# Scores of a token with itself by an elementwise product and a matmul with ones, in a gated linear attention kernel

## The chip, the cores and the metric

The kernel runs on one core of a Trainium2 chip. Its time is the device time of one execution in microseconds (us), the median of several runs. The core's engines are TensorE (PE, and PEld for its loading of stationary weights), VectorE (DVE), ScalarE (ACT), GpSimd (POOL) and SyncE (SP), each working through a list of its own in the order in which the program gives it, with semaphores between them.

## The reference

Inputs: q, k, v, f_logit of shape 4 x 8 x 768 x 48 (batch, heads, tokens, width), and the weights of two feed-forward parts. All of it is fp32.

```python
f = 1.0 / (1.0 + np.exp(-f_logit))
for t in range(S):
    state = f[:, :, t, :, None] * state + np.einsum('bhd,bhe->bhde', k[:, :, t], v[:, :, t])
    y[:, :, t] = np.einsum('bhd,bhde->bhe', q[:, :, t], state)
```

The output of this attention (8 heads side by side, 768 tokens x 384) goes through a low-rank mix over the tokens and `u + relu(u @ w_ch1) @ w_ch2` (first part), and then `h = relu(x @ w_in)`, a gated convolution over three tokens, and `@ w_out` (second part).

In a block of 64 tokens, the attention is a matrix of scores. The score of query token t with key token s up to t is the sum over the 48 channels of q[t] k[s] and of the gates of the tokens s+1 to t. With itself (s = t) a token has no gate: the score is q[t] . k[t].

## The kernel before

The unit of the attention is a duo: 256 tokens of one batch, all 8 heads, held as channels x tokens in `q_t`, `k_t` and `gates` (112 partitions: one head of a pair in rows 0 to 47, the other in 64 to 111; 1024 columns). There are three duos for each of the 4 batches, 12 in all. A duo's scores are 32 blocks of 64 x 64.

Scores are made in seven steps. `DIAG` comes first: 32 matmuls of k with q (line 547), each in one quadrant of the array (the pair `par`, `ch`), of which only the diagonal is kept: VectorE copies it under `diag_mask` into `scores` (line 949). Between, VectorE multiplies the whole of q by the gates (line 991). Then come levels 0 to 5. Level l gives the scores of query tokens whose bit l is one with key tokens whose bit l is zero, in the same group of 2 x 2^l tokens: 32 matmuls with 32 moving columns (line 566), and a masked copy (line 955, `take_scores`; ScalarE does it in the last levels). After its matmuls, a level multiplies half of q by products of gates on VectorE (line 1002) and half of k on GpSimd (line 1123, at level 0 by the gates themselves). GpSimd also makes the products of gates for levels 1 and 2 (line 1126, `pairs_ready`), VectorE the later ones. Steps T, U and Y close a duo: transposed k, the update of the state, the output, copied to `x` by ScalarE.

A list written out by `schedule()` sets the order on each engine. The three duos of batch 0 run first, interleaved among themselves, each with its own buffers, before any feed-forward work: I call this the prologue (0 to about 81 us). After it the duos of batch b+1 are spread over the 40 slots of the feed-forward work of batch b, one step a slot at first. A slot of the first part (0 to 23) holds `first1` (nine matmuls, lines 681 to 683), the step of a duo, and `second1` (nine matmuls, lines 700 to 705) of two slots before; slots 0 and 1 have no `second1`, but transposes and mix matmuls (lines 660 and 666). DIAG stands in slots 0, 11 and 22, level 0 in 1, 12 and 23. In a slot's list, the residual of `first1` (`r_lo`, line 1044, on VectorE) stands ahead of the duo's step. In batch 0's slots GpSimd also splits the weights (line 1133), two pieces a slot, ahead of the duo's step.

## Time and profile before

| | before |
|---|---|
| median of 3 runs | 738.42 us (738.24 to 738.48) |
| profiled execution | 738.63 us, of which its span is 736.7 us |
| PE busy | 704.6 us, 96% of the span |
| PEld busy | 664.4 us |
| DVE busy | 441.7 us |
| ACT busy | 246.4 us |
| POOL busy | 289.7 us |

The span is from the first to the last instruction of the profiled execution; 1.9 us of its time lie around it. An engine is busy while an instruction of its own runs. A row of the timeline gives start and duration in us, engine, line, operation, what is written and what is read, and how many instructions were merged (x64); in brackets the idle time of the engine before it and who ended it. A fp32 matmul is two records of the trace: line 547 has 32 matmuls and x64 in a duo. The time from one record's start to the next one's is shorter than a record, since they are pipelined.

### The profile page before, as it was taken

How to read it: one execution, taken by the hardware profiler on the slowest of the kernel's cores; microseconds unless marked ns; L12 is line 12 of the kernel's file. 1: busy time of each engine (PE TensorE's matmuls, PEld its weight loads, DVE VectorE, ACT ScalarE, POOL GpSimd, SP SyncE). 2: the span in 40 equal slices, each digit the busy share in tenths (PEclk: the TensorE clock that was granted, in tenths of full speed). 3: DMA queues.
4: the chain of work that ended last, by engine and by line, in shares of the span. 5: the costliest groups of instructions: out<-in, count | busy, mean ns of one | idle time of the engine just before them, and what ended most of it. 6: DMA issues, size and time to landing. Idle time of an engine off the chain costs nothing.

```text
span 736.7 us, 23832 instructions
## 1 busy us (share of the span) xinstructions
PE 704.6 (96%) x10748; PEld 664.4 (90%) x10748; DVE 441.7 (60%) x706; ACT 246.4 (33%) x504; POOL 289.7 (39%) x262
## 2 busy tenths in 40 slices
PE   3888989999999999999999999999999999999998
PEld 3787789989999899999999889999999889999997
DVE  6895474573898464464598655365489832121875
ACT  1034524342236322212245431213134542121453
POOL 4862597691453234062253225145055311030432
PEclk9999999999999999999999999999999999999999
DMA  8331353412001110100201200110000000000000
GB/s 202 100 91 40 109 148 91 127 57 66 24 3 54 45 55 23 46 24 24 67 2 46 53 34 25 41 49 24 23 2 2 34 33 1 1 1 0 1 33 32
DMA packets 24293, 33.75 MB, mean 46 GB/s; under 512 B 5152, under 2 KB 17184, under 8 KB 24192
## 3 DMA queue, kind: packets, MB, share of 16 engines
q1 hardware_dynamic: 23184, 30.46, 15.3%
q10 hardware_dynamic: 1008, 1.77, 1.0%
q8 instruction: 84, 1.38, 0.8%
q14 instruction: 17, 0.14, 0.1%
HBM read 27.50 MB, written 4.72 MB: 44 GB/s over the span
## 4 chain that ended last, share of the span: by engine, by line
PE 72%; DVE 18%; issue 4%; ACT 3%; POOL 1%; DMA 1%; ACTq 0%; DVEq 0%; POOLq 0%
PE acc L700 8%; PE hb L681 7%; PE att L566 7%; PE hb L682 7%; PE hb L683 6%; PE acc L701 6%; PE acc L705 6%; DVE conv L1074 5%; DVE q_t L1002 3%; PE att L612 3%; DVE conv L1071 3%; PE acc L739 2%; PE hb L649 2%; PE acc L740 2%; DVE conv L1058 2%
## 5 line engine op out<-in xcount | busy, mean ns | idle before, releaser
L1044 DVE SCALAR_TENSOR_TENSOR r_lo<-hb,r_hi 128x386 fp32r<-128x386 f32 (+1 forms) x96 | 53.5, 557 | 193.2 <-ACT r_hi L864 193.2
L864 ACT ACTIVATE r_hi<-hb 128x386 fp32r<-128x386 f32 (+1 forms) x96 | 47.2, 492 | 260.1 <-PE hb L683 260.1
L1160 POOL TENSOR_TENSOR r_lo<-conv,r_hi 128x384 fp32r<-128x384 f32 x64 | 61.7, 964 | 168.6 <-ACT r_hi L879 168.6
L700 PE MATMUL acc<-r_hi,w_ch_hi 128*128 128x386 f32 (+1 forms) x288 | 103.8, 360 | 0.0
L1123 POOL TENSOR_TENSOR k_t<-k_t,blocks 112x512 f32<-112x512 f32 x60 | 81.5, 1361 | 55.2 <-PE att L566 45.0
L681 PE MATMUL hb<-u_hi,w_ch_hi 128*128 128x386 f32 (+1 forms) x288 | 98.3, 341 | 0.2 <-DVE r_lo L1044 0.2
L682 PE MATMUL hb<-u_hi,w_ch_lo 128*128 128x386 f32 (+1 forms) x288 | 97.5, 339 | 0.0
L701 PE MATMUL acc<-r_hi,w_ch_lo 128*128 128x386 f32 (+1 forms) x288 | 97.3, 338 | 0.0
L683 PE MATMUL hb<-u_lo,w_ch_hi 128*128 128x386 f32 (+1 forms) x288 | 96.9, 337 | 0.0
L566 PEld LDWEIGHTS att<-q_t,k_t 48*64 48x64 f32 (+3 forms) x3840 | 59.3, 134 | 25.6 <-issue 23.9
L1074 DVE SCALAR_TENSOR_TENSOR conv<-hb,convw,conv 128x384 f32<-128x384 f32 x128 | 79.1, 618 | 4.5
L1123 POOL TENSOR_TENSOR k_t<-k_t,gates 112x512 f32<-112x512 f32 x12 | 23.3, 1942 | 140.5 <-PE att L566 140.2
L566 PE MATMUL att<-q_t,k_t 48*64 48x32 f32 (+3 forms) x3840 | 66.0, 219 | 11.3 <-DVE scores L949 3.4
L1002 DVE TENSOR_TENSOR q_t<-q_t,blocks 112x512 f32<-112x512 f32 x60 | 68.3, 1138 | 7.2 <-PE att L566 5.0
L739 PE MATMUL acc<-w_out_hi,r_hi 128*128 128x384 f32 x192 | 67.6, 352 | 1.3 <-ACT ostage L902 1.3
L705 PE MATMUL acc<-r_lo,w_ch_hi 128*128 128x386 f32 (+1 forms) x288 | 66.1, 338 | 0.0
L720 PE MATMUL hb<-u_hi,w_in_hi 128*128 128x388 f32 x192 | 65.4, 341 | 0.0
L722 PE MATMUL hb<-u_lo,w_in_hi 128*128 128x388 f32 x192 | 65.0, 338 | 0.0
L721 PE MATMUL hb<-u_hi,w_in_lo 128*128 128x388 f32 x192 | 64.8, 338 | 0.0
L740 PE MATMUL acc<-w_out_lo,r_hi 128*128 128x384 f32 x192 | 64.7, 337 | 0.0
L700 PEld LDWEIGHTS acc<-r_hi,w_ch_hi 128*128 128x128 f32 x288 | 54.2, 188 | 2.6
L873 ACT ACTIVATE conv<-conv 128x384 f32<-128x384 f32 x64 | 33.7, 527 | 65.3 <-DVE conv L1074 65.3
(134 smaller groups left out, 1343.4 us busy)
## 6 DMA issues: line engine op xcount, KB each, us to landing
v_p<-in_vn_dram SPq DMA_DIRECT2D x12, 384.0 KB, 3.6
out_dram<-ostage SPq DMA_DIRECT2D x24, 192.0 KB, 2.0
q_t<-in_qT_dram SPq DMA_DIRECT2D x21, 192.0 KB, 3.6
k_t<-in_kT_dram SPq DMA_DIRECT2D x21, 192.0 KB, 3.5
gates<-in_fT_dram SPq DMA_DIRECT2D x21, 192.0 KB, 3.5
ostage<-in_w_ch_dram SPq DMA_DIRECT2D x14, 192.0 KB, 2.8
conv<-in_w_ch_dram SPq DMA_DIRECT2D x10, 192.0 KB, 2.9
ostage<-in_w_out_dram SPq DMA_DIRECT2D x5, 192.0 KB, 2.5
```

The source lines that it names most:

```text
L566: mm = pe.matmul(banks[o:o + left, par, g * C:g * C + 32], k[rows, first:first + left], moving, start=True, stop=True, skip_group_check=True)
L681: pe.matmul(o, wh[:, t, ws], u_hi[:, t, cols], start=(t == 0), stop=False)
L682: pe.matmul(o, wl[:, t, ws], u_hi[:, t, cols], start=False, stop=False)
L683: mm = pe.matmul(o, wh[:, t, ws], u_lo[:, t, cols], start=False, stop=(t == CT - 1))
L700: pe.matmul(o, wh[:, j, ws], r_hi[:, s, 0:width], start=(j == 0), stop=False)
L701: pe.matmul(o, wl[:, j, ws], r_hi[:, s, 0:width], start=False, stop=False)
L705: mm = pe.matmul(o, wh[:, j, ws], r_lo[:, s, 0:width], start=False, stop=(j == N1 - 1))
L739: pe.matmul(o, r_hi[:, s, ts], wh[:, j, :], start=(j == 0), stop=False)
L740: pe.matmul(o, r_hi[:, s, ts], wl[:, j, :], start=False, stop=False)
L1002: nc.vector.tensor_tensor(view, view, block_product(products(gates[i], blocks[i], st), c, 0), ALU.mult).then_inc(q_ready, 1)
L1074: nc.vector.scalar_tensor_tensor(out=c, in0=hid[:, tap + 1:HALF + tap + 1], scalar=convw[:, j, tap:tap + 1], in1=c, op0=ALU.mult, op1=ALU. ...
L1123: nc.gpsimd.tensor_tensor(view, view, block_product(ends, c, 1), ALU.mult).then_inc(k_ready, 1)
```

## The change

The step DIAG is replaced by a step EVEN at the same places of the list, with no work on PE.

- EVEN on VectorE: the product of q and k for even tokens alone (512 columns) goes into the unused second half of `blocks`; then q of the even tokens is multiplied by their gates. On GpSimd, the multiplication of k by the gates (before: after level 0's matmuls) and the first products of gates stand here, and wait for that product (`selves_ready`) and the gates.
- Level 0 on PE: first 4 matmuls of ones (48 x 64) with the product, 256 moving columns each, one in each quadrant; they put the sum over the channels in every row of the first 32 columns of a block. Then the 32 matmuls of k with odd q go to the other 32 columns. k is gated by then in its even tokens and q is not yet gated in its odd ones, so that the same matmul gives an odd token's score with itself and with the even token before it.
- Level 0 on VectorE: odd q is multiplied by the products of two gates, and one masked copy of 1024 columns takes all, in place of line 949's (1024) and level 0's of line 955 (512). It reads its source with a step: neighbours in `scores` lie 32 columns apart in PSUM.
- The constants: `ones` is set, and `first_mask` is made in three small steps. The loads of the third duo wait for the even q of the first (`q_ready`) and no longer for `level_done` of DIAG.

```diff
-                if st == DIAG:
-                    pe.wait_ge(loaded_q[q_of(n)], 32 * q_use(n))
-                    pe.wait_ge(loaded_k[i], 32 * set_use(n))
+                if st == EVEN:
+                    return
+                if st == 0:
+                    if n == 0:
+                        pe.wait_ge(ones_ready, 1)
+                    pe.wait_ge(selves_ready, selves(n))
                     if set_before(n) is not None:
                         pe.wait_ge(x_copied, copies(set_before(n)))
...
-                                mm = pe.matmul(banks[o:o + C, par, g * C:(g + 1) * C], k[rows, first:first + C],
-                                               q[rows, first:first + C], start=True, stop=True, skip_group_check=True)
-                    mm.then_inc(level_done, 1)
-                elif st < LEVELS:
+                    sums = self_products(n).rearrange("p (g h m) -> p g h m", h=2, m=32)
+                    for par, ch in QUADRANTS:
+                        rows, o = slice(C * par, C * par + D), C * ch
+                        pe.matmul(banks[o:o + C, par, :].rearrange("p (g x) -> p g x", x=C)[:, :, 0:32], ones[rows, :],
+                                  sums[rows][:, :, ch, :], start=True, stop=True, skip_group_check=True)
+                if st < LEVELS:
                     c = 1 << st
-                    pe.wait_ge(q_ready, levels(n, st - 1))
+                    pe.wait_ge(k_ready, gated(n, max(st - 1, 0)))
                     if st > 0:
-                        pe.wait_ge(k_ready, gated(n, st - 1))
...
             def take_scores(n, st):
...
+                if st == 0:
                     nc.vector.copy_predicated(
-                        sc[:].rearrange("p (g t) -> p g t", t=C),
-                        diag_mask[:].rearrange("p (o t) -> p o t", o=1).broadcast_to([P, BLOCKS, C]),
-                        from_psum).then_inc(level_taken, 1)
+                        sc[:].rearrange("p (g m two) -> p g m two", g=BLOCKS, two=2),
+                        first_mask[:].rearrange("p (o m two) -> p o m two", o=1, two=2).broadcast_to([P, BLOCKS, 32, 2]),
+                        from_psum.rearrange("p g (two m) -> p g m two", two=2)).then_inc(level_taken, 1)
...
-                if st == DIAG:
+                if st == EVEN:
+                    dve.wait_ge(loaded_q[q_of(n)], 32 * q_use(n))
+                    dve.wait_ge(loaded_k[i], 32 * set_use(n))
+                    even, even_k = split_blocks(q, 1)[:, :, 0, 0], split_blocks(k_t[i][0:PR, :], 1)[:, :, 0, 0]
+                    nc.vector.tensor_tensor(self_products(n), even, even_k, ALU.mult).then_inc(selves_ready, 1)
                     dve.wait_ge(gates_ready, n + 1)
-                    dve.wait_ge(level_done, levels(n, DIAG))
-                    nc.vector.tensor_tensor(q, q, gates[i][0:PR, :], ALU.mult).then_inc(q_ready, 1)
+                    dve.wait_ge(selves_ready, selves(n))
+                    nc.vector.tensor_tensor(even, even, split_blocks(gates[i][0:PR, :], 1)[:, :, 0, 0],
+                                            ALU.mult).then_inc(q_ready, 1)
+                elif st == 0:
+
+                    dve.wait_ge(pairs_ready, paired(n, 0))
+                    dve.wait_ge(level_done, levels(n, 0))
+                    odd = split_blocks(q, 1)[:, :, 1, 0]
+                    nc.vector.tensor_tensor(odd, odd, products(gates[i], blocks[i], 1), ALU.mult).then_inc(q_ready, 1)
...
-                pool.wait_ge(level_done, levels(n, st))
                 if st == 0:
+                    pool.wait_ge(selves_ready, selves(n))
                     pool.wait_ge(gates_ready, n + 1)
                 else:
+                    pool.wait_ge(level_done, levels(n, st))
                     pool.wait_ge(k_ready, gated(n, st - 1))
```

VectorE, slots 11 and 12 of batch 1 (the step DIAG or EVEN, then level 0). Before:

```order
266 L991 TENSOR_TENSOR q_t<-q_t,gates 112x1024 [waits level_done,gates_ready]
267 L949 COPY_PREDICATED scores<-diag_mask,att 128x1024
268 L1044 SCALAR_TENSOR_TENSOR r_lo<-hb,r_hi 128x382 [waits r_hi_ready]
269 L1002 TENSOR_TENSOR q_t<-q_t,gates 112x512 [waits q_ready,level_done]
270 L955 COPY_PREDICATED scores<-masks,att 128x512 [waits level_taken]
```

The same place now:

```order
269 L1019 TENSOR_TENSOR blocks<-q_t,k_t 112x512 [waits loaded_k0,loaded_q0]
270 L1022 TENSOR_TENSOR q_t<-q_t,gates 112x512 [waits selves_ready,gates_ready]
271 L1082 SCALAR_TENSOR_TENSOR r_lo<-hb,r_hi 128x382 [waits r_hi_ready]
272 L1029 TENSOR_TENSOR q_t<-q_t,blocks 112x512 [waits level_done,pairs_ready]
273 L976 COPY_PREDICATED scores<-first_mask,att 128x1024
```

The step needs nothing of PE any more, one masked copy is gone, and level 0's multiplication waits for GpSimd's products of gates.

GpSimd at the start of the program, three duos interleaved (the rows with `gates` are the first gating of k and the first products of a duo). Before:

```order
13 L1123 TENSOR_TENSOR k_t<-k_t,gates 112x512 [waits gates_ready,level_done,cleared_k]
14 L1126 TENSOR_TENSOR blocks<-gates 112x512
15 L1123 TENSOR_TENSOR k_t<-k_t,blocks 112x256x2 [waits pairs_ready,k_ready,level_done]
16 L1126 TENSOR_TENSOR blocks<-blocks 112x256
17 L1123 TENSOR_TENSOR k_t<-k_t,gates 112x512 [waits gates_ready,level_done]
18 L1126 TENSOR_TENSOR blocks<-gates 112x512
19 L1123 TENSOR_TENSOR k_t<-k_t,blocks 112x128x4 [waits pairs_ready,k_ready,level_done]
20 L1123 TENSOR_TENSOR k_t<-k_t,blocks 112x256x2 [waits pairs_ready,k_ready,level_done]
21 L1126 TENSOR_TENSOR blocks<-blocks 112x256
22 L1123 TENSOR_TENSOR k_t<-k_t,blocks 112x64x8 [waits merged_ready,k_ready,level_done]
23 L1123 TENSOR_TENSOR k_t<-k_t,gates 112x512 [waits gates_ready,level_done]
```

The same place now:

```order
13 L1163 TENSOR_TENSOR k_t<-k_t,gates 112x512 [waits gates_ready,selves_ready,cleared_k]
14 L1166 TENSOR_TENSOR blocks<-gates 112x512
15 L1163 TENSOR_TENSOR k_t<-k_t,gates 112x512 [waits gates_ready,selves_ready]
16 L1166 TENSOR_TENSOR blocks<-gates 112x512
17 L1163 TENSOR_TENSOR k_t<-k_t,blocks 112x256x2 [waits pairs_ready,k_ready,level_done]
18 L1166 TENSOR_TENSOR blocks<-blocks 112x256
19 L1163 TENSOR_TENSOR k_t<-k_t,blocks 112x128x4 [waits pairs_ready,k_ready,level_done]
20 L1163 TENSOR_TENSOR k_t<-k_t,gates 112x512 [waits gates_ready,selves_ready]
21 L1166 TENSOR_TENSOR blocks<-gates 112x512
22 L1163 TENSOR_TENSOR k_t<-k_t,blocks 112x256x2 [waits pairs_ready,k_ready,level_done]
```

The second duo's pair of instructions moved ahead of the first duo's level 1, the third duo's ahead of the second duo's level 1.

## Rows read from the trace of the kernel before

**Rows 1.** The page: busy time of each engine; TensorE's granted clock, 40 slices.

```profile
PE 704.6 (96%) x10748; PEld 664.4 (90%) x10748; DVE 441.7 (60%) x706; ACT 246.4 (33%) x504; POOL 289.7 (39%) x262
...
PEclk9999999999999999999999999999999999999999
```

**Rows 2.** Waits of PE from 78 us on: total us, times, longest.

```profile
PE att L566 <- DVE scores L955: 2.8, 2, 1.5
PE att L566 <- POOL k_t L1123: 1.4, 3, 0.5
```

**Rows 3.** Timeline of PE, slots 11 to 13 of batch 1.

```profile
306.81 0.34 PE L683 MATMUL hb<-u_lo,w_ch_hi 128*128 128x386 f32 x1
307.08 1.16 PE L547 MATMUL att<-q_t,k_t 48*64 48x64 f32 x64
308.17 0.44 PE L700 MATMUL acc<-r_hi,w_ch_hi 128*128 128x386 f32 x1
308.45 0.34 PE L701 MATMUL acc<-r_hi,w_ch_lo 128*128 128x386 f32 x1
...
311.54 1.14 PE L566 MATMUL att<-q_t,k_t 48*64 48x32 f32 x64
...
315.98 1.14 PE L566 MATMUL att<-q_t,k_t 48*64 48x32 f32 x64
```

**Rows 4.** Timeline of DVE, the same slots.

```profile
307.71 0.56 DVE L1044 SCALAR_TENSOR_TENSOR r_lo<-hb,r_hi 128x386 fp32r<-128x386 f32 x1 [5.12 <-ACT r_hi L864]
308.38 1.23 DVE L991 TENSOR_TENSOR q_t<-q_t,gates 112x1024 f32<-112x1024 f32 x1
309.52 1.31 DVE L949 COPY_PREDICATED scores<-diag_mask,att 128x1024 f32<-128x1024 uint8 x1
...
312.74 0.69 DVE L1002 TENSOR_TENSOR q_t<-q_t,gates 112x512 f32<-112x512 f32 x1
313.35 1.35 DVE L955 COPY_PREDICATED scores<-masks,att 128x512 f32<-128x512 uint8 x1
```

**Rows 5.** Timeline of POOL, the same slots.

```profile
312.79 2.03 POOL L1123 TENSOR_TENSOR k_t<-k_t,gates 112x512 f32<-112x512 f32 x1 [22.54 <-PE att L566]
314.79 1.03 POOL L1126 TENSOR_TENSOR blocks<-gates 112x512 f32<-112x512 f32 x1
```

**Rows 6.** Timeline of PE, the mix matmuls of batch 0.

```profile
77.52 2.82 PE L649 MATMUL hb<-x,mixu 128*96 128x384 f32 x8
80.18 0.60 PE L660 MATMUL hb<-ident_r,x 128*128 128x128 f32 x4
```

**Rows 7.** Timeline of DVE: level 2's masked copy of a duo.

```profile
148.28 0.70 DVE L955 COPY_PREDICATED scores<-masks,att 128x512 f32<-128x512 uint8 x1
```

**Rows 8.** Timeline of PE, slots 0 to 2 of batch 1.

```profile
261.21 1.16 PE L547 MATMUL att<-q_t,k_t 48*64 48x64 f32 x64
...
265.11 1.14 PE L566 MATMUL att<-q_t,k_t 48*64 48x32 f32 x64
...
268.49 1.14 PE L566 MATMUL att<-q_t,k_t 48*64 48x32 f32 x64 [0.47 <-POOL k_t L1123]
```

**Rows 9.** Timeline of DVE: slot 2 of batch 0; then slot 0 of batch 1.

```profile
94.14 3.46 DVE L1002 TENSOR_TENSOR q_t<-q_t,blocks 112x512 f32<-112x512 f32 x1 [0.52 <-PE att L566]
...
262.51 1.23 DVE L991 TENSOR_TENSOR q_t<-q_t,gates 112x1024 f32<-112x1024 f32 x1
```

**Rows 10.** Timeline of all engines in the prologue.

```profile
15.27 1.99 PE L547 MATMUL acc<-q_t,k_t 48*64 48x64 f32 x64
...
24.48 1.50 POOL L1123 TENSOR_TENSOR k_t<-k_t,gates 112x512 f32<-112x512 f32 x1
...
29.16 1.66 POOL L1123 TENSOR_TENSOR k_t<-k_t,blocks 112x512 f32<-112x512 f32 x1 [0.57 <-PE acc L566]
...
33.36 1.54 POOL L1123 TENSOR_TENSOR k_t<-k_t,gates 112x512 f32<-112x512 f32 x1 [0.38 <-PE hb L566]
...
37.82 1.93 PE L566 MATMUL hb<-q_t,k_t 48*64 48x32 f32 x64
```

More of the change, by code:

```diff
@@ L37 @@
 QUADRANTS = [(par, ch) for par in range(2) for ch in range(2)]
-DIAG, T, U, Y = -1, LEVELS, LEVELS + 1, LEVELS + 2
-STEPS = list(range(DIAG, Y + 1))
+EVEN, T, U, Y = -1, LEVELS, LEVELS + 1, LEVELS + 2
+STEPS = list(range(EVEN, Y + 1))
 PAD = 2
@@ L305, in bass_gla_lowrank_mix_ffn_gated_conv_ffn @@
         convw = sb("convw", [P, N2, 3])
+        ones = sb("ones", [P, C])
         ident_r = sb("ident_r", [P, P], F32R)
```

72 lines of the change are left out of this document (42 added, 30 removed).

## The prediction

> **What bounds the kernel now.** I read the page first: PE is busy for 704.6 of 736.7 us [rows 1], so after the prologue a microsecond taken from PE is a microsecond of the time, unless PE then waits for somebody. Next come the waits of PE from 78 us on. Those that touch the steps of this change are small: 2.8 us for VectorE's masked copies and 1.4 us for GpSimd's gating of k, three times up to 0.5 us [rows 2]. The reader is to see two things: PE's own work is the bound, and in slot 2 of a batch the wait for GpSimd is already there. Last come the timelines of the slots that change.
>
> The own time of the profiled execution is 738.63 us, 736.7 of span and 1.9 around it; the sum is made against 738.63, and the median is 0.2 lower. A measurement of this kernel can tell 0.2%, some 1.5 us.
>
> **1. What leaves PE.** DIAG's 64 records start at 307.08, and the next large matmul at 308.17 [rows 3]. The large matmul before started at 306.81, and one follows another in 0.17 to 0.18 us, so PE was free for the next at 306.99: the group takes 1.18 us. The first large matmul behind it takes 0.28 us to the next in place of 0.18 [rows 3], which adds 0.10. A duo so gives back 1.28 us; of nine duos behind the prologue that would be 11.5 us.
>
> **2. What comes to PE.** Four matmuls of 256 columns, eight records. The nearest row is the mix: eight fp32 records of 384 columns start at 77.52, and the next group at 80.18, 0.333 us each [rows 6], so 0.22 us for 256 columns. If the four quadrants run side by side the group takes 2 x 0.22 = 0.44 us, one after another 8 x 0.22 = 1.78. DIAG decides: its 64 records of 64 columns would by the same rate take 64 x 0.055 = 3.5 us one after another, and took 1.16 [rows 3], three at least at a time. So it is between 0.44 and 1.78/3 = 0.59 us; I take 0.45. It stands directly ahead of level 0's small matmuls, so no second change to and from large matmuls is paid.
>
> A rule bears on it: the Trainium skill, page "TensorE: Matmul & The Clock Gate", section "Part 3: Packing small matmuls", has four row-packed tiles run 3.07 times as fast as one by one. By that the group would take 0.58 us, and the nine duos 1.2 us more than my sum where PE is what is late.
>
> **3. The new wait of level 0, slots 11 and 22 (six duos).** Level 0 now waits for GpSimd's gating of k, which waits for VectorE's product. The chain, with the times of rows 4: `r_lo` starts at 307.71 and is over at 308.27; the product of 512 columns is of the kind of the 0.69 us row (512 columns, sources with a step of two), so 308.95. VectorE goes straight on with even q, another 0.69. GpSimd's gating took 2.03 us where VectorE's 0.69 us instruction had started just ahead of it, 312.74 against 312.79 [rows 4, 5], and 1.50 where it had not [rows 10]. The pair of instructions meets in the same way now, so I take 2.03: k is ready at 311.0. PE meanwhile has `second1` and `first1`; before, level 0 started at 311.54 [rows 3], so without DIAG PE gets there at 310.26, does the ones until 310.71, and waits until 311.03. Level 0 starts 0.5 us earlier than before, and not 0.83. Six duos: **-3.0 us**. If GpSimd gets in first (1.50) it is -0.83 each and -5.0; if the ones take 0.59 nothing changes, since k is what is late.
>
> The products of gates end 1.03 us [rows 5] behind the gating, at 312.0, before level 0's matmuls do (312.2): VectorE's new wait for them costs nothing.
>
> **4. The masked copy.** It has 1024 columns, contiguous in the target, as line 949's with 1.31 us [rows 4]. Level 0's old copy took 1.35 us for 512 columns [rows 4], level 2's 0.70 [rows 7]. Mask and source are read alike in both, and only the target differs (single words against runs of four); this penalty goes away. But the new source steps by 32 columns at every element, which no row shows. Bounds: 1.31, and 2.4, twice the rate of 1.31, as the penalty of the target was a factor of two. Nothing excludes either end; I take the middle, 1.85.
>
> The Trainium skill, page "Vector Engine (DVE) Microarchitecture Reference", section "5.2 Measured stream behaviour on trn2", gives 1.73 ns a column where one source hops at every element against 1.054 contiguous. By that the copy takes 1.9 us; no row here shows such a source.
>
> In slots 12 and 23 the copy is hidden: level 0's matmuls end at about 312.1, multiplication and copy take 0.65 + 1.85, so 314.7; level 1 would start at 315.98 [rows 3] less 0.5. Even 2.4 us fit, by 0.2.
>
> **5. Slots 0 to 2 (three duos).** Here no `second1` stands between. In batch 1, VectorE's L991 started at 262.51, held by DIAG [rows 9]; the product can start at 262.35, so k is ready at 262.35 + 0.69 + 0.05 + 2.03 = 265.1. Before, level 0 started at 265.11 [rows 8]. PE would be there at 263.83 + 0.45 = 264.3, and waits: all of step 1 is eaten, gain 0. Its work ends at 266.3. Between it and level 1 stand only `first1`'s 1.6 us, and before, level 1 waited for GpSimd until 268.49 [rows 8]. That wait goes, and VectorE's is next: 266.35 + 0.6 + 1.85 + 0.1 = 268.9, so **+0.45 us** in batches 1 and 2 (-0.1 with 1.31, +1.0 with 2.4): +0.9.
>
> In batch 0, GpSimd's weight pieces lie between. Before, VectorE's multiplication at 94.14 took 3.46 us [rows 9] in place of 0.69, while pieces and gating ran on GpSimd, and level 2 waited for 1.5 us of it [rows 2]. Gating and products now stand two pieces earlier, so about two pieces of work are over before that point. I take back 1.2 of the 1.5 us, less the 0.45: **-0.8** (bounds -1.5 and +1.5, if the new multiplication by the products falls into such a stretch instead).
>
> **6. The prologue.** PE does not bound it; the three engines take turns. There the same L547 group takes 1.99 us, not 1.16 [rows 10, 3], with a granted clock shown as full in both [rows 1]; the ones I put at 0.9. I listed the starts with the rows' durations. First duo: gates at 11.0, GpSimd 2.0, level 0's 1.9 us from 13.0, VectorE 0.7 + copy, level 1 at 17.7 with 1.85. The second duo's pair on GpSimd (1.5 + 1.0) comes ahead of the first's level 1. Further on the third duo's pair, which stood at 33.36, goes ahead of the second's level 1, which stood at 29.16 [rows 10]: that stays where it was (29.4 with a copy of 1.31, 31.2 with 2.4), and GpSimd is free of the pair behind it. The third duo's level 1, before at 37.82 [rows 10], then starts at 35.2 with 1.31, and at 38 with 2.4 at most. With 1.85: **-1.3 us** (+0.3 to -2.6).
>
> **7. What costs nothing.** The loads of the third duo start some 1.5 us later (the even q of the first duo in place of its DIAG), ahead of ACT's second sigmoid and SP's later loads; the third duo's q is first needed at about 27 us. `ones` and the mask steps are 0.5 us of VectorE before the first gates are ready (11.0). If q and k were late, the product would be, by as much.
>
> **Sum:** -3.0 + 0.9 - 0.8 - 1.3 = -4.2; 738.63 - 4.2 = 734.4 us, as a median 734.2.
>
> **The rivals.**
> A. The stepped source is free: copy 1.31. Steps 5 and 6 become -0.2, -1.2 and -2.6, sum -7.0: 731.4. For it: a step of two costs nothing in the 0.69 us rows. Against: these stay within neighbouring words.
> B. The stepped source halves the rate: copy 2.4. Sum -3.0 + 2.0 + 0 - 0.3 = -1.3: 737.1. For it: the factor of two that the masked copy shows at its target.
> C. The chain through VectorE and GpSimd becomes the bound of level 0. Each 0.1 us that it is longer than 2.8 us costs 0.1 in all nine duos. It decides from 0.47 us on (no gain); if GpSimd loses to both new multiplications and not to one, it is 0.69 longer: -4.2 + 6.2 = +2.0: 740.4. For it: the 3.46 us row [rows 9] and the 0.5 us at 312.79. Against: the product must be over before GpSimd may start, so it can meet one only.
> D. Part of the copy's stepped read is far dearer than a factor of two. From 2.65 us it shows in slots 13 and 24 too; slower than before from about 2.9. Taken with C.
>
> **How the numbers follow.** Forecast 0.45, A 0.22, B 0.18, C and D 0.15. The forecast's own range is 732 to 737. With A and B, the ends of steps 5 and 6, the range is 730.5 to 739.5, which leaves C's tail and a luckier GpSimd out. Faster by over 0.2% (under 736.9): 0.9 of the forecast, all of A, a third of B: 0.67. Slower: C and D, 0.15. Within: 0.18.
>
> **What would show it.** The new copy's duration (1.3, 1.85 or 2.4); eight records of ones within 0.45 us; level 0 of slots 12 and 23 waiting 0.3 us for GpSimd's k, of slot 1 some 0.8; level 1 of slot 2 waiting for VectorE's copy; the gating of k at 2.0 or 1.5 us; the end of the prologue's attention 1.3 us earlier. The prediction is wrong if ones run one after another (+1.3 each), if another engine's pace in the prologue undoes its part, or if the copy is outside 1.3 to 2.4.

## The result, and the profile after

Eight executions of the changed kernel have a median of **735.36 us** (733.25 to 737.34), the kernel before on the same chip 738.66 us (736.91 to 742.12): a ratio of 0.9928, interval 0.9906 to 0.9951. That ratio is not the quotient of the two medians, which is 0.9955: by the medians the change is worth 3.3 us, by the ratio some 5.3 (3.6 to 6.9). The forecast was 734.2 us, with a range of 730.5 to 739.5. The profiled execution took 736.56 us, 734.8 of them span, against 738.63 and 736.7 before.

The page of the changed kernel, busy time of each engine and the granted clock in 40 slices:

```profile
PE 699.3 (95%) x10076; PEld 657.7 (90%) x10076; DVE 446.1 (61%) x709; ACT 246.3 (34%) x504; POOL 286.3 (39%) x262
...
PEclk9999979999999999999999999999999999999999
```

PE's busy time fell by 5.3 us [rows 1] and the span by 1.9. The clock row has what the row of before does not: one slice, the sixth, at 7 tenths. The waits of PE from 78 us on (total us, times, longest) are the next thing to read:

```profile
PE hb L700 <- DVE r_lo L1082: 2.9, 2, 2.8
PE att L585 <- DVE scores L976: 1.9, 2, 0.9
...
PE att L585 <- DVE scores L982: 1.3, 1, 1.3
PE att L585 <- POOL k_t L1163: 0.8, 3, 0.5
```

One wait of 2.8 us is new. The waits for masked copies are 3.2 us (1.9 and 1.3) and were 2.8, those for GpSimd's k are 0.8 and were 1.4 [rows 2]. The new wait stands in batch 0, behind level 0 of slot 1 and ahead of the first matmul of slot 2. The timelines of PE, VectorE and GpSimd there (start, duration, and in brackets the idle time before and who ended it):

```profile
87.00 0.66 PE L567 MATMUL att<-blocks,ones 48*64 48x256 f32 x8
88.13 1.14 PE L585 MATMUL att<-q_t,k_t 48*64 48x32 f32 x64 [0.47 <-POOL k_t L1163]
92.05 0.69 PE L700 MATMUL hb<-u_hi,w_ch_hi 128*128 128x386 f32 x1 [2.78 <-DVE r_lo L1082]
92.53 0.53 PE L701 MATMUL hb<-u_hi,w_ch_lo 128*128 128x386 f32 x1
...
95.25 1.93 PE L585 MATMUL att<-q_t,k_t 48*64 48x32 f32 x64
...
102.27 1.14 PE L585 MATMUL att<-q_t,k_t 48*64 48x32 f32 x64
```

```profile
86.60 4.92 DVE L1022 TENSOR_TENSOR q_t<-q_t,gates 112x512 f32<-112x512 f32 x1
91.44 0.55 DVE L1082 SCALAR_TENSOR_TENSOR r_lo<-hb,r_hi 128x386 fp32r<-128x386 f32 x1
```

```profile
86.58 1.50 POOL L1163 TENSOR_TENSOR k_t<-k_t,gates 112x512 f32<-112x512 f32 x1 [0.63 <-DVE blocks L1019]
88.03 1.04 POOL L1166 TENSOR_TENSOR blocks<-gates 112x512 f32<-112x512 f32 x1
89.03 1.95 POOL L1173 TENSOR_TENSOR w_ch_lo<-ostage,w_ch_hi 128x384 fp32r<-128x384 f32 x2
90.93 2.41 POOL L1173 TENSOR_TENSOR w_ch_lo<-conv,w_ch_hi 128x384 fp32r<-128x384 f32 x2
```

The reader is to see a chain. GpSimd starts its gating of k at 86.58, VectorE its multiplication of even q at 86.60. GpSimd has no gap in its work until 93.3, and VectorE's instruction, 0.69 us of work in other places, lasts 4.92 us. `r_lo` of slot 1 stands behind it, and PE cannot reuse a bank of `hb` until `r_lo` has read it. After this wait the large matmuls follow one another every 0.32 us and not every 0.18 (92.53 to the next at 92.85), and level 1 takes 1.93 us and not 1.14. That is the clock, by the windows of the same stretch (columns: PE, PEld, DVE, ACT, POOL busy, PEclk, DMA share, GB/s):

```profile
82.00:90.00 8.00, 6.76 (x102) 5.75 (x102) 6.24 (x6) 6.11 (x13) 6.53 (x8) 1.00 0.46 126
90.00:101.00 11.00, 8.96 (x85) 8.45 (x86) 7.58 (x9) 1.30 (x3) 7.06 (x8) 0.54 0.57 143
```

1.00 is the level of 2.4 GHz; 0.54 means that nearly all of this stretch ran at 1.2. The clock's own records put the half level at 90.85 to 101.09 us. In the kernel before the same stretches have 1.00.

The places for which the prediction had reckoned look otherwise. Slots 11 and 12 of batch 1, PE, then VectorE, then GpSimd (against [rows 3 to 5]):

```profile
311.84 0.66 PE L567 MATMUL att<-blocks,ones 48*64 48x256 f32 x8
312.32 1.08 PE L585 MATMUL att<-q_t,k_t 48*64 48x32 f32 x64
```

```profile
309.78 0.68 DVE L1019 TENSOR_TENSOR blocks<-q_t,k_t 112x512 f32<-112x512 f32 x1
310.57 2.04 DVE L1022 TENSOR_TENSOR q_t<-q_t,gates 112x512 f32<-112x512 f32 x1
312.53 0.54 DVE L1082 SCALAR_TENSOR_TENSOR r_lo<-hb,r_hi 128x382 fp32r<-128x382 f32 x1
313.55 0.69 DVE L1029 TENSOR_TENSOR q_t<-q_t,blocks 112x512 f32<-112x512 f32 x1 [0.47 <-POOL blocks L1166]
314.16 1.32 DVE L976 COPY_PREDICATED scores<-first_mask,att 128x1024 f32<-128x1024 uint8 x1
```

```profile
310.54 1.52 POOL L1163 TENSOR_TENSOR k_t<-k_t,gates 112x512 f32<-112x512 f32 x1 [18.70 <-DVE blocks L1019]
312.02 1.49 POOL L1166 TENSOR_TENSOR blocks<-gates 112x512 f32<-112x512 f32 x1
```

GpSimd's gating took 1.52 us, and it is VectorE's multiplication that was held, for 2.04 us. Level 0 follows the ones without a wait. The masked copy of 1024 columns with a stepped source took 1.32 us. In slots 0 to 2 of batch 1 (against [rows 8]):

```profile
265.42 0.66 PE L567 MATMUL att<-blocks,ones 48*64 48x256 f32 x8
266.24 1.14 PE L585 MATMUL att<-q_t,k_t 48*64 48x32 f32 x64 [0.16 <-POOL k_t L1163]
...
270.08 1.14 PE L585 MATMUL att<-q_t,k_t 48*64 48x32 f32 x64 [0.94 <-DVE scores L976]
```

**Where the time went.** The prologue differs from execution to execution by some microseconds, so I compare from the eight matmuls of the mix [rows 6] to the end of the span. Before: 736.7 - 77.52 = 659.2 us. After, the group starts at 76.35: 734.8 - 76.35 = 658.4. Within this stretch the even step of each duo is a mark (VectorE's L991 before, L1019 after), its time counted from the mix:

```
                  batch 0            batch 1                    batch 2                    end
step of slot      11       22        0        11       22       0        11       22
before            56.92    105.42    184.99   230.86   278.04   357.74   403.62   450.76   659.2
after             61.21    108.84    187.57   233.43   279.73   358.63   404.50   450.73   658.4
after - before    +4.29    +3.42     +2.58    +2.57    +1.69    +0.89    +0.88    -0.03    -0.8
```

Four statements come out of this table. Until slot 11 of batch 0 the changed kernel has lost 4.3 us. Each of the six duos of slots 11 and 22 then gives back 0.7 to 0.9 us, 5.0 together. Slots 0 to 2 of batches 1 and 2 give 0.0. The rest of the 1.9 us, 1.2, lies ahead of the mix.

### The profile page after: what moved, and what is told of

The parts are those of the page before. It is cut to its first block, busy times and chain, and to the rows that moved or that the text cites. A ratio compares the mean times of both kernels' runs of the same rounds, so it can differ in the third digit from the quotient of the medians.

```text
span 734.8 us, 22489 instructions
## 1 busy us (share of the span) xinstructions
PE 699.3 (95%) x10076; PEld 657.7 (90%) x10076; DVE 446.1 (61%) x709; ACT 246.3 (34%) x504; POOL 286.3 (39%) x262
## 4 chain that ended last, share of the span: by engine, by line
PE 69%; DVE 21%; issue 5%; ACT 3%; DMA 1%; POOL 1%; ACTq 0%; DVEq 0%; POOLq 0%
PE acc L719 8%; PE hb L700 7%; PE acc L720 7%; PE acc L724 6%; PE hb L701 6%; PE hb L702 6%; PE att L585 5%; DVE conv L1112 5%; DVE q_t L1040 4%; PE att L631 3%; DVE conv L1109 3%; PE hb L668 2%; PE acc L758 2%; DVE conv L1096 2%; PE acc L759 2%
## 5 line engine op out<-in xcount | busy, mean ns | idle before, releaser
L1040 DVE TENSOR_TENSOR q_t<-q_t,blocks 112x512 f32<-112x512 f32 x60 | 66.3, 1105 | 4.7 <-PE att L585 3.4
L759 PE MATMUL acc<-w_out_lo,r_hi 128*128 128x384 f32 x192 | 64.6, 337 | 0.0
L1163 POOL TENSOR_TENSOR k_t<-k_t,gates 112x512 f32<-112x512 f32 x12 | 18.5, 1542 | 113.6 <-DVE blocks L1019 108.7
L700 PEld LDWEIGHTS hb<-u_hi,w_ch_hi 128*128 128x128 f32 x288 | 54.9, 191 | 3.9 <-DVE r_lo L1082 3.3
```

Of the source, the lines that this page charges most:

```text
L700: pe.matmul(o, wh[:, t, ws], u_hi[:, t, cols], start=(t == 0), stop=False)
L759: pe.matmul(o, r_hi[:, s, ts], wl[:, j, :], start=False, stop=False)
L1040: nc.vector.tensor_tensor(view, view, block_product(products(gates[i], blocks[i], st), c, 0), ALU.mult).then_inc(q_ready, 1)
L1163: nc.gpsimd.tensor_tensor(view, view, block_product(ends, c, 1), ALU.mult).then_inc(k_ready, 1)
```

## The experiments

Two theories stood against each other as to the 4.3 us. **P**: GpSimd's run of gating, products and four weight pieces back to back holds VectorE, so `r_lo` and with it PE is late, and the clock falls behind the wait. **F**: the fall of the clock and the loss belong to the new order of PE's work and come whatever VectorE does. Since executions scatter by 2 us, the table gives medians with the ratio to the kernel before on the same chip (its medians there were 739.7 to 740.1), and beside them the stretch from the mix to the end in the profiled execution, which repeats better (658.4 in both traces of the changed kernel). The last column is PE's longest wait in slots 1 to 6 of batch 0; one of 1.3 us, ahead of level 4 of a later duo, and one of 0.7 for `rstack` ahead of slot 0 are in every kernel.

```
kernel                     median   ratio (interval)         mix starts  stretch  longest wait, slots 1-6
before                     738.66                            77.52       659.2    1.5
before_again               740.54   0.9991 (0.9959-1.0024)   79.98       660.8    1.5
changed kernel             735.36   0.9928 (0.9906-0.9951)   76.35       658.4    2.8
after_again                735.41   0.9945 (0.9927-0.9964)   77.65       658.4    2.8
e1_even_late               734.05   0.9923 (0.9896-0.9950)   76.15       658.2    3.3
e2_late_one_duo            736.15   0.9945 (0.9924-0.9965)   76.70       657.8    3.3
e3_no_ones                 735.49   0.9944 (0.9920-0.9969)   78.32       658.4    2.7
e4_dummy_diag              745.08   1.0073 (1.0046-1.0101)   78.02       662.6    1.4
e5_pieces_after_level1     734.25   0.9926 (0.9900-0.9953)   74.91       658.2    1.9
e5w_gpsimd_waits           733.58   0.9917 (0.9889-0.9945)   74.22       655.6    2.3
e6_even_a_slot_earlier     728.04   0.9845 (0.9812-0.9878)   73.21       650.5    0.9
e7_even_earlier_no_waits   730.85   0.9870 (0.9836-0.9904)   76.29       653.0    1.9
e8_two_copies              737.26   0.9955 (0.9927-0.9982)   78.02       657.8    2.0
e9_second1_ahead           727.72   0.9831 (0.9797-0.9864)   76.79       649.2    0.2
```

### The changed kernel again

No edit; a second trace.

> The changed kernel once more, beside the experiments on one chip. In its first profile VectorE's multiplication of the even q in slot 0 of batch 0 took 4.92 us beside GpSimd's work, PE then waited 2.78 us for the residual behind it, and the granted clock was half from 90.9 to 101.1 us. If that belongs to the kernel, the same stretch shows again: a wait of 2 to 3 us and a clock of 0.5 for about 10 us, and the time is 3 us (0.4%) under the kernel before. If it was an accident of one execution, clock and wait are absent and the profiled time is some 6 us lower.

Measured: 735.41 us, and batch 0 again has the multiplication of 4.93 us, the wait of 2.8 us and the half clock for 10.2 us. The mean granted clock of an execution is 0.993 in all eight executions of the changed kernel and in seven of eight here (one 0.995), where the kernel before has 1.0 in seven of fifteen on this chip and 0.986 to 0.999 in the others. The same stretch in both traces, and the same clock in nearly every execution, say that the event belongs to the kernel and not to one execution.

### Even q's multiplication moved behind level 0

```diff
                 elif st == 0:
 
                     dve.wait_ge(pairs_ready, paired(n, 0))
+                    if late(n):
+                        even = split_blocks(q, 1)[:, :, 0, 0]
+                        nc.vector.tensor_tensor(even, even, split_blocks(gates[i][0:PR, :], 1)[:, :, 0, 0],
+                                                ALU.mult).then_inc(even_ready, 1)
                     dve.wait_ge(level_done, levels(n, 0))
```

(and the same instruction taken out of the step EVEN): in e1 `late(n)` is true for all duos, in e2 for the one whose even step stands in slot 0 of batch 0. In e1 the loads of the third duo wait for the first product, `selves_ready`, in place of `q_ready`.

> In all twelve duos VectorE multiplies the even q by the gates only after GpSimd's products of gates (in level 0's step), not in the step EVEN; the loads of the third duo wait for the first product. Theory 1 (the even multiplication meets GpSimd's work, holds up the residual of the first part in slot 0 of batch 0, PE waits and its clock falls): wait and clock fall go, 2.8 + 5 us less than the changed kernel, about 728. Rival (the clock fell for another reason, or the prologue's change of pace is what is missing): the time stays within 1.5 us of the changed kernel's, 734 to 737, and the clock falls again.

> The same edit for the one duo whose EVEN stands in slot 0 of batch 0; the other eleven are as in the changed kernel. Theory 1: nearly the whole gain of the edit in all duos comes from this one, 6 to 8 us under the changed kernel. Rival: the even multiplication costs about 0.5 us in each duo, and this run gains under 1 us.

Measured: neither gained what theory 1, which is P in its first form, had promised; the stretch is 0.2 to 0.6 us shorter. Timeline of e1 in batch 0, GpSimd, VectorE and PE:

```profile
88.85 1.98 POOL L1184 TENSOR_TENSOR w_ch_lo<-ostage,w_ch_hi 128x384 fp32r<-128x384 f32 x2
88.92 2.46 DVE L1036 TENSOR_TENSOR q_t<-q_t,gates 112x512 f32<-112x512 f32 x1 [0.95 <-POOL blocks L1177]
90.79 2.85 POOL L1184 TENSOR_TENSOR w_ch_lo<-conv,w_ch_hi 128x384 fp32r<-128x384 f32 x2
91.30 1.48 DVE L1040 TENSOR_TENSOR q_t<-q_t,blocks 112x512 f32<-112x512 f32 x1
...
94.14 1.93 PE L591 MATMUL att<-q_t,k_t 48*64 48x32 f32 x64 [3.28 <-DVE scores L982]
```

The hold has not gone but moved: now the pieces meet the multiplication 2.5 us later, counted from the mix, `r_lo` is in time, the copy is late instead, and PE waits 3.3 us in front of level 1. So the question to ask of such an edit is which of VectorE's instructions with two inputs in SBUF meets the run of pieces. Before the change this run had a gap: between pieces 9 and 10 GpSimd stood idle for 0.79 us, until level 0 was done, and VectorE's multiplication of level 0 started in it and took 0.69 us. The pair of instructions now stands ahead of the pieces and closes it.

### DIAG's matmuls put back without use

The changed kernel with as many matmuls as DIAG had (64 records per duo, ones with ones) in the step EVEN, written into banks that level 0 overwrites.

> The changed kernel with 32 matmuls of ones (48 x 64, 64 moving columns) put back on PE in the step EVEN of every duo; their results are overwritten. It prices what left PE. Theory (the nine duos behind the prologue give back 0.8 to 0.9 us each where nothing is waited for): each of the six duos in slots 11 and 22 costs 1.28 us more, those in slot 0 of batches 1 and 2 about 0.8 (PE's wait of 0.47 for GpSimd goes), together 9 us; in batch 0 the longer slot may spare PE the long wait and the clock fall, 5 to 8 us back. So between 736 and 745. Rival (PE's work is not what sets the time after the change): within 2 us of the changed kernel, with the clock fall in place.

Measured: 745.08 us, +9.7 against after_again and slower than before. In the trace the stretch grew by 4.2 us. By the marks of the table above, each of the six duos of slots 11 and 22 takes 1.27 to 1.31 us more than in the changed kernel, and the way from slot 0 to slot 11 of batches 1 and 2 0.4 more, together 8.6; up to slot 11 of batch 0 it is 4.4 less, for the half clock behind 78 us does not come. This confirms step 1 of the prediction (1.28 a duo). It also shows that the loss in batch 0 ate what had been taken from PE. Why the half clock does not come there, two rows tell:

```profile
88.25 3.03 DVE L1035 TENSOR_TENSOR q_t<-q_t,gates 112x512 f32<-112x512 f32 x1
91.81 0.44 PE L713 MATMUL hb<-u_hi,w_ch_hi 128*128 128x386 f32 x1 [0.30 <-DVE r_lo L1095]
```

PE waits 0.30 us and not 2.78. Counted from the mix PE is there 0.6 us later than in the changed kernel, and `r_lo` starts 1.9 us earlier (13.19 and 15.09), since VectorE's multiplication takes 3.03 us and not 4.92. VectorE and GpSimd have the same lists in both kernels: the list alone does not fix how long the hold is.

The profiled execution was the fastest of the six, 742.38 us, 4.6 above that of after_again: 4.2 in the stretch and 0.4 ahead of the mix. The other 5 us between the medians stand in no trace; three groups of DIAG at the prologue's 1.99 us [rows 10] would be 6.0.

### GpSimd's pieces moved, or made to wait

```diff
-            for task in ORDER:
+            held_back = [("piece", i) for i in range(8, 12)]
+            own = [t for t in ORDER if t not in held_back]
+            at = own.index(("att", DUOS, 1)) + 1
+            own[at:at] = held_back
+            for task in own:
```

> On GpSimd's own list the four weight pieces of slots 1 and 2 of batch 0 (numbers 8 to 11) stand behind its work for level 1 of the fourth duo; nothing else is changed. Theory P (VectorE is held because GpSimd runs the gating of k, the products and four pieces back to back): the even q multiplication of batch 0 takes 2.0 us in place of 4.9, PE's wait of 2.8 us for r_lo goes, the clock does not fall, and 4 to 6 us go: 729.5 to 731.5. But six pieces then follow one another from about 93 us on, and the multiplication of q for level 2 may be held by them for some 2 us. Rival F (the clock falls and PE waits whatever GpSimd does in this place, since the ones and level 0 have come earlier): 734 to 736 as in the changed kernel.

```diff
                 elif kind == "piece":
+                    if task[1] == 8:
+                        pool.wait_ge(q_ready, scaled(DUOS, EVEN))
+                    if task[1] == 10:
+                        pool.wait_ge(q_ready, scaled(DUOS, 0))
                     piece(task[1])
```

> The changed kernel with two waits on GpSimd, in batch 0 alone: piece 8 waits until even q is multiplied, piece 10 until odd q is. The pieces keep their places. Theory P: VectorE gets in behind GpSimd's gating or products of gates, at 2.0 to 3.0 us in place of 4.9; PE's wait for r_lo is under 1 us and the clock does not fall: 729.5 to 732. Rival F: 734 to 736.

Measured: 734.25 and 733.58 us, in both cases above what P had promised (731.5 and 732 at most). The multiplication of 4.9 us falls to 2.0 in both, and the wait for `r_lo` to 0.2, as P says, though nothing is changed on PE. But e5 gained little, as `first1` of slot 3 needs piece 8, which now comes late:

```profile
95.25 0.41 PE L700 MATMUL hb<-u_hi,w_ch_hi 128*128 128x386 f32 x1 [1.79 <-POOL w_ch_lo L1173]
```

The clock is at half behind this wait, for 3.4 us. And in front of level 5, in slot 6, PE waits 1.9 us for a masked copy; the multiplication ahead of that copy took 4.42 us beside pieces and gating on GpSimd. In e5w the timelines of VectorE and PE are

```profile
84.49 2.03 DVE L1022 TENSOR_TENSOR q_t<-q_t,gates 112x512 f32<-112x512 f32 x1
...
87.84 2.07 DVE L1029 TENSOR_TENSOR q_t<-q_t,blocks 112x512 f32<-112x512 f32 x1
```

```profile
91.26 1.40 PE L585 MATMUL att<-q_t,k_t 48*64 48x32 f32 x64 [2.30 <-DVE scores L976]
```

so pieces 8 and 9 hold the multiplication of odd q by 1.4 us, and level 1 waits for the copy; half clock for 3.4 us. The stretch is 2.8 us shorter than after's. P is right as to the hold, and short as to the remedy: as long as four pieces stand in slots 1 and 2, something of VectorE's meets them.

### The even step one slot earlier

```diff
-                    at.setdefault(s, []).append((n + j, st))
+                    if (j, st) != (0, EVEN):
+                        at.setdefault(s, []).append((n + j, st))
...
+                if s == 0 and b + 1 < B:
+                    order.append(("att", DUOS * (b + 1), EVEN))
                 order.append(("first1", b, s))
```

for all engines, for the first duo of each batch; in e6 with the two waits of e5w, in e7 without.

> e5w_gpsimd_waits, and in addition the step with the even tokens of the first duo of each batch stands ahead of the batch's first first1 in place of behind it, for all engines. In slot 1 of the three batches level 0 waited some 0.5 us for GpSimd's k: with the pair 1.3 us earlier this wait goes. If PE is the bound behind it: 1 to 1.5 us less than e5w. If level 1's wait for the masked copy (0.9 us twice) is what is late in slot 2, it shrinks as well, as level 0 comes earlier: up to 2.5 less. Rival: the product and the multiplication then stand ahead of r_lo of the first slot on VectorE, and r_lo is late by as much: no gain or +0.5 us.

> e6_even_a_slot_earlier without the two waits on GpSimd; what is left is the changed kernel with the even step of the first duo of each batch ahead of first1. Theory P (it is GpSimd's run of gating, products and pieces back to back, met by VectorE's even q multiplication, that makes r_lo late): the pair now stands where GpSimd waits for a weight piece, so VectorE gets in or is held ahead of a slot that needs nothing of it; but odd q's multiplication may meet pieces 8 to 11 and be held up to 4 us. 727.5 to 731, the clock does not fall or for 3.4 us. Rival F (the waits on GpSimd made the gain of e6): 733 or more, with the clock at half for some 10 us.

Measured: 728.04 us with the waits, more than expected (5.5 us under e5w, where 1 to 2.5 were forecast), and 730.85 without, as expected: stretches of 650.5 and 653.0, against 658.4. PE waits and granted clock in e6:

```profile
PE att L588 <- DVE scores L979: 1.7, 3, 0.9
...
PE att L588 <- POOL k_t L1166: 0.2, 1, 0.2
```

```profile
90.00:101.00 11.00, 11.00 (x179) 10.41 (x178) 7.38 (x10) 2.62 (x6) 10.28 (x9) 1.00 0.74 202
```

The even step stands where VectorE and GpSimd do not meet, level 0's wait for k goes from 0.8 us to 0.2, the waits for copies shrink, and the clock stays up (1.00, PE busy for all 11 us). Of the 5.1 us by which e6's stretch is shorter than e5w's, 2.5 are the waits for the copy and 0.6 those for k; 2.0 are left, of which e5w's half clock of 3.4 us can account for 1.7. Without the waits on GpSimd, e7 has in batch 0

```profile
89.11 2.16 DVE L1032 TENSOR_TENSOR q_t<-q_t,blocks 112x512 f32<-112x512 f32 x1 [1.00 <-PE att L588]
```

```profile
92.63 1.16 PE L588 MATMUL att<-q_t,k_t 48*64 48x32 f32 x64 [1.85 <-DVE scores L979]
```

and half clock for 3.4 us. F is refuted: in e5 and e5w PE's list is the changed kernel's, and the wait for `r_lo` is gone; in e6 level 0 comes earlier still, and the clock does not fall at all.

### The ones left out

```diff
-                    for par, ch in QUADRANTS:
+                    for par, ch in QUADRANTS if n < DUOS else []:
```

The even tokens' scores with themselves are missing in the nine duos behind the prologue.

> The changed kernel without the four matmuls with ones for the nine duos behind the prologue (the even tokens' scores with themselves are missing from its sums). It prices step 2. By the steps of the prediction: 0.45 us less in each of the six duos of slots 11 and 22 only if k is there in time; GpSimd's gating of k takes 1.5 us here, so about 0.35 to 0.45 each, 2.1 to 2.7 in all, and nothing in slots 0 to 2, where PE waits for k anyway: 732.5 to 733.5. If four quadrants do not run side by side: 6 x 1.0 and more, under 730. If the waits for k fill what goes: no change.

Measured: 735.49 us and a stretch of 658.4, no change. The third answer of the expectation held:

```profile
PE att L585 <- POOL k_t L1163: 4.7, 9, 1.1
...
314.29 1.14 PE L585 MATMUL att<-q_t,k_t 48*64 48x32 f32 x64 [0.30 <-POOL k_t L1163]
```

The waits for k rose from 0.8 us in three duos to 4.7 in nine, 3.9 us more; nine groups of ones at 0.44 would be 4.0. From the even step of slot 0 to that of slot 11 batch 1 took 45.86 us with the ones and without. Counted from the mix, level 0 of slot 12 of batch 1 starts at 235.97 us in both kernels. So k is what is late in **all nine** duos, and the ones lie in front of it: it arrives at the moment at which PE is done with them.

### The one copy undone into two

```diff
-                    nc.vector.copy_predicated( ... 1024 columns ... ).then_inc(level_taken, 1)
+                    for half in range(2):
+                        copied = nc.vector.copy_predicated( ... [:, :, :, half] ... 512 columns ... )
+                    copied.then_inc(level_taken, 1)
```

on the base of e6.

> e6_even_a_slot_earlier with the one masked copy of 1024 columns undone into two of 512: even places of the target, then odd places, each from 32 columns in a run. It prices the single copy. Each half writes single words two apart, which took 1.35 us for 512 columns in the kernel before, so VectorE's work is 2.6 to 2.7 us in place of 1.3. In slot 2 of the three batches PE already waits for this copy (1.7 us in three): +1.3 each, +3.9. In slots 12, 13, 23 and 24 it is hidden by second1 and two first1 (0.9 us of room by the timeline of the kernel before): up to +0.4 each, +2.4 at most. In the prologue up to +2. Sum +4 to +8: 732 to 736. Rival (the target's single words cost nothing and the copy is bound by its columns): 0.7 us each, no change, 728.

Measured: 737.26 us, above the 732 to 736 expected; 9.2 over e6, and the stretch 7.3 longer. The waits for this copy grew by 3.9 us (from 1.7 to 5.6), as reckoned; what the expectation left out are two stretches at half clock of 3.4 us, 1.7 us each. That makes the 7.3. Its copies, and level 1 in batch 1:

```profile
L980 DVE COPY_PREDICATED scores<-first_mask,att 128x512 f32<-128x512 uint8 x20 | 24.5, 1330 | 0.0
...
269.01 1.23 PE L588 MATMUL att<-q_t,k_t 48*64 48x32 f32 x64 [1.52 <-DVE scores L980]
```

512 columns into single words take 1.33 us, as in [rows 4], and the 1024 of the single copy 1.31: the rate is set by the target's pattern. In this batch the wait of 1.52 us is followed by 3.4 us at half clock, likewise in batch 0, behind 2.0 us; but not in batch 2, behind 1.53 us at the same place, and not in the kernel before behind its longest wait, 1.5 us [rows 2]. The copy was the point of the change, and worth more than a rate can tell, since the price is a wait of PE plus the clock behind it.

### `second1` ahead of the levels

```diff
+            if behind:
+                order.append(("second1", b, q))
             for n, st in at.get(s, []):
                 order.append(("att", n, st))
...
-                order.append(("second1", b, q))
+                if not behind:
+                    order.append(("second1", b, q))
```

with `behind` true in the slots in which the first duo of a batch has levels 1 to 5; on the base of e6.

> e6_even_a_slot_earlier with second1 ahead of levels 1 to 5 in the slots of the first duo of each batch, in place of behind them, for all engines. PE's waits of 0.9, 0.4 and 0.4 us for the masked copy in slot 2 should go, if the later levels keep their distance: 1.5 to 1.7 us less than e6. Rival: second1 needs r_lo of the slot before, and then waits for it: no gain.

Measured: the three waits for level 0's masked copy are gone (0.9, 0.4 and 0.4 us in e6), and the stretch is 1.3 us shorter, 649.2, near the 1.5 to 1.7 expected; the medians, 727.72 and 728.04, do not tell this apart. It has the lowest median of these kernels, 1.7% under the kernel before (0.9831, 0.9797 to 0.9864), and 7.7 us under the change as it stood.

### The kernel before again

> The kernel before, unchanged, for a second trace of it: it tells how far the start of the first mix group (73.0 us in the first trace) scatters from execution to execution, and so how much of the difference of two profiled spans is prologue. The other traces so far have it from 69.7 to 73.0 us, with no change in their code ahead of it. If the prologue's gain of some 1.2 us is real, it is at 72 to 74 us here; if it is scatter, anywhere from 70 to 74. From there to the end: 663.7 us within 0.5 if what lies behind the prologue repeats.

Measured: 740.54 us. Both numbers of the expectation missed: the first mix matmul of all starts at 75.1 us (70 to 74 expected), and from it to the end are 665.6 us (663.7). The eight mix matmuls start 2.5 us later than in the first trace, and the stretch is 1.6 us longer:

```profile
79.98 2.82 PE L649 MATMUL hb<-x,mixu 128*96 128x384 f32 x8
```

The 1.6 us are no work of PE: counted from the mix, the last matmul ends at 655.6 us in the first trace and at 655.5 in this one, and at 654.8 in both traces of the changed kernel.

The start of the mix goes with TensorE's clock. It rose at 77.3 us here and at 74.5 in the first trace. That it was at half before is told by the weight loads of one shape (kernel before, in the prologue and later; changed kernel, in the half-clock stretch of batch 0), for the view shows 1.00 up to the first record of the clock:

```profile
L547 PEld LDWEIGHTS acc<-q_t,k_t x64: 222/223/224, 15.2 to 16.8; 48*64 48x64 f32 x64
L547 PEld LDWEIGHTS att<-q_t,k_t x512: 129/135/136, 133.1 to 527.9; 48*64 48x64 f32 x171
L585 PEld LDWEIGHTS att<-q_t,k_t x64: 177/223/223, 95.2 to 96.8; 48*64 48x64 f32 x64
```

223 ns belong to the 1.2 GHz level and 135 ns to 2.4, and all traces have the 223 ns in the prologue until the clock rises. The mean start of the mix is 78.8 us in the two traces of before, and 76.0, from 73.2 to 78.3, in the nine whose prologue is the changed one (after, after_again, e2, e3, e5, e5w, e6, e7, e9). In two of these nine, e5w and e6, the clock rose at 64.6 and 60.6 us, in the other seven at 71.8 to 76.3, with the mix 2.0 to 3.2 us behind; these seven have a mean of 76.7.

## Why the prediction was right, point by point

The time fell within the range and 1.2 us from the number, but that it came so near was luck: batch 0 was 5.1 us worse than reckoned, slots 11 and 22 were 2.0 better, slots 0 to 2 of the other batches 0.9, and the prologue up to 1.5.

1. **What leaves PE, 1.28 us a duo** (step 1): held: put back in e4, such a group costs 1.27 to 1.31 us a duo. Six duos gave 5.0 us; 1.28 less the ones' 0.45 is 0.83 each, 5.0 in all.
2. **The ones, 0.45 us** (step 2): held in size. Level 0 starts 0.48 us behind the first of them (311.84 to 312.32), so the quadrants run side by side; the rule on packing in the Trainium skill (page "TensorE: Matmul & The Clock Gate", section "Part 3: Packing small matmuls"), by which it would be 0.58 as an estimate, was 0.1 too slow here. That they *cost* 0.45 on the path was wrong: e3 shows that they cost nothing.
3. **Level 0 waits for GpSimd in slots 11 and 22, -3.0** (step 3): the failed step in size. I took the gating of k at 2.03 us, held by VectorE as in [rows 5]; behind the prologue it took 1.50 to 1.52, since GpSimd started 0.03 us ahead of VectorE (310.54 and 310.57), and VectorE's instruction is the one that was held, 2.04 us. The prediction named this case ("if GpSimd gets in first (1.50) it is -0.83 each and -5.0"), and -5.0 is what came. For all that it was the right chain: by e3, k is late in all nine duos, by just what the ones cover.
4. **The masked copy, 1.85 us** (step 4): wrong, 1.28 to 1.32 us; a source in PSUM that steps by 32 columns costs nothing, and the lower bound (rival A) was the value. The Trainium skill's 1.73 ns a column (page "Vector Engine (DVE) Microarchitecture Reference", section "5.2 Measured stream behaviour on trn2") was measured on streams in SBUF. It gives an estimate of 1.8 us and does not carry over to this read from PSUM: 1.31 us for 1024 columns are 1.28 ns each. The upper bound was mis-sized as well, twice 1.31 being 2.6 and not 2.4; and rival B's sum should have taken step 6 at its +0.3, not -0.3, so -0.7 and 737.7.
5. **Slots 0 to 2 of batches 1 and 2, +0.9** (step 5): 0.0, and with the copy at 1.31 the step itself gave -0.2. The order of what is late was right: level 0 waits for k (0.16 us and more behind the ones), level 1 for the copy (0.94).
6. **Batch 0, -0.8, bounds -1.5 and +1.5** (step 5): the failed step in sign, outside its bounds: **+4.3**. I reckoned that gating and products now stand two pieces earlier, and that two pieces of work are over before VectorE's multiplication. I had not asked what stands right *ahead* of the pieces now: without level 0's wait between them, GpSimd has one run of six instructions, and the multiplication that starts together with the first of them stays held through four (it ends at 91.52, and the second piece at 90.98). Price by the rows: PE's wait 2.8; the half clock over nine matmuls (3.2 us and not 1.7, from 92.05 to 95.25), level 1 (1.9, not 1.1), `second1` (3.1, not 1.7) and three more matmuls (0.95, not 0.5), together 4.1; less the 1.5 us that level 2 waited before, 0.5 for level 1's k, and 0.3 that level 0 came earlier. That is 4.6; the start of level 2 moved by 25.92 - 21.45 = 4.5. Nothing in the sum provided for a clock that falls behind a wait.
7. **The prologue, -1.3** (step 6): -1.2 between the two first traces; by the means of all traces -2.8, or -2.0 without e5w and e6, where the step had -2.6 with a copy of 1.31. With two traces of before that differ by 2.5 us this is no more than "of this size". Step 6 also read the granted clock as full in the prologue; the weight loads of 223 ns show half. The durations it listed came from the prologue's own rows, so its sum does not suffer from this.

With the measured terms: -5.0 (slots 11 and 22), 0.0, +4.3 (batch 0), and -1.2 to -2.8 (prologue) = -1.9 to -3.5, against 738.66 - 735.36 = 3.3 us of the medians and some 5.3 by the ratio: the parts are known better than the whole. Without the event in batch 0 the sum would lie near rival A's -7.0 (slots 11 and 22 with the prologue alone are -6.2 to -7.8), an estimate; no run shows just this. e6 and e7, which are rid of most of the event, stand 7.8 and 5.4 us below after_again in their stretches, part of which is the wait for k that they take away as well.

Rival C (the chain through VectorE and GpSimd bounds level 0) was at the edge: the chain is what is late everywhere, but at 0.0 us over the ones. Rivals B and D fell with the copy's duration.

What stays open is where VectorE gets in. In ten duos of the changed kernel, and in e5 and e5w in batch 0 too, it did so after the gating (2.02 to 2.05 us, and the products then took 1.49); in batch 0 of the changed kernel not even after the products (4.92, in three traces of three: after, after_again, e3), and in e4 after the products (3.03), with the same lists of VectorE and GpSimd as in the changed kernel. No run tells what decides it. The Trainium skill (page "SBUF — State Buffer", section "SBUF: two separate sides") has whoever starts first keep the pair of ports for the whole instruction. The 2.03 us agree with it (1.34 us of hold for a gating of 1.50). So does the kernel before in slot 0 of batch 0, where VectorE got in between two weight pieces:

```profile
86.88 1.32 DVE L991 TENSOR_TENSOR q_t<-q_t,gates 112x1024 f32<-112x1024 f32 x1
86.11 3.92 POOL L1133 TENSOR_TENSOR w_ch_lo<-ostage,w_ch_hi 128x384 fp32r<-128x384 f32 x3
```

Here VectorE lost 0.09 us against [rows 4], and it was the second of the three pieces that took 2.00 us, the others 1.0 each. The 4.92 us over four instructions of GpSimd go beyond what the page says.

## What to carry to other kernels

When an edit takes a wait out of an engine's list, write down what that engine now does without a gap, and which instructions of its neighbour meet this run; the wait may have been the gap through which the neighbour got in. Two waits on GpSimd and one step moved by a slot (e6) were worth 7.4 us of the medians, twice the 3.3 of the change itself. Price a wait of PE not by its length alone: here waits of 1.5 to 3.3 us were followed by 3.4 to 10.2 us at half clock, and 2.8 us of wait cost 6.9. And when a term is removed and nothing happens, as with the ones, look at the wait that has grown by just that much: it names the next bound.

## What the runs showed of the hardware

- A two-input multiplication of VectorE, 0.69 us alone, took 2.02 to 2.05 us behind one GpSimd instruction, 2.1 to 2.5 behind two weight pieces (e5w, e7, e1), 3.03 in e4, 3.46 us in the kernel before [rows 9], and 4.92 us over the first four of six GpSimd instructions without a gap. `r_lo` and the masked copies, which read one input from PSUM, kept their 0.56 and 1.31 us beside the same pieces.
- The masked copy of 1024 columns from PSUM takes 1.31 us with a source in single steps of 32 columns, as with a contiguous one. Into single words two apart, 512 columns take 1.33 us, as long as 1024 contiguous ones.
- PE's clock fell to the 1.2 GHz level behind waits of 2.8 us (for 10.2 us; 2.7 in e3), 3.3 (6.8), 2.3, 2.0, 1.9, 1.8 and 1.5 us (3.4 each). Behind waits of 0.9, 1.3 and 1.4 us it did not, nor behind the 1.5 us of the kernel before in both its traces, a wait of 1.53 us of e8 in batch 2, and one of 1.9 us of e5 in slot 6: the length of the wait alone does not tell.
- The same weight load takes 223 ns at the 1.2 GHz level and 135 at 2.4. In the prologue it takes 223 ns in all traces until the clock rises (60.6 to 77.3 us), where the view, ahead of its first record of the clock, shows 1.00.
